# The last tile's gate on three column groups, and five first loads issued from ScalarE's queue

## The reference: windowed attention, a cosine layer, a routed expert layer

```python
# q, k, v: (4, 8, 576, 64); heads 0-3 see a window of 32 keys, heads 4-7 every 4th of 128
scores = where(mask, q @ k.T / 8, -1e9);  attn = softmax(scores);  x = attn @ v   # -> (2304, 512)
h = x @ w_in;  y = (h * cos(h)) @ w_out                        # (512, 2048), (2048, 512)
logits = y @ w_gate
noisy = logits + log1p(exp(y @ w_noise)) * noise               # (2304, 8)
# top 2 of 8 experts per row, softmax weights over the two
out[rows of e] += weight * (relu(y[rows] @ w1[e]) @ w2[e])      # (8, 512, 1024), (8, 1024, 512)
```

## Time and profile before

| | |
|---|---|
| runs | 1009.29, 1009.43, 1011.7 us; median 1009.43 us |
| profiled execution | 1009.55 us, span 1007.8 us |
| PE | 992.0 us busy, 98% of the span |
| DVE, ACT, POOL | 575.2, 445.8, 354.9 us busy |
| DMA | 101252 packets, 99.60 MB |

### The profile page before, as it was taken

The page is one execution under the profiler, slowest core; times in us unless marked ns, Lnnn a source line. Parts: engine busy times, 40 slices in busy tenths (PEclk is TensorE's granted clock), DMA queues, the critical chain, the costliest instruction groups (busy, mean ns, idle before and its releaser), DMA issues. The chain is left out here.

```text
span 1007.8 us, 17738 instructions
## 1 busy us (share of the span) xinstructions
PE 992.0 (98%) x6176; PEld 877.2 (87%) x6176; DVE 575.2 (57%) x1189; ACT 445.8 (44%) x1091; POOL 354.9 (35%) x349
## 2 busy tenths in 40 slices
PE   7999999999999999999999999999999999999998
PEld 5878898888889889889888888999898989999896
DVE  4888766576576576576676754434344444424322
ACT  5989665453454544534547333333132323323111
POOL 2656786222222222222231355143241425133241
PEclk9999999999999999999999999999999999999999
DMA  9787356000000000005006154434353533434130
GB/s 203 178 177 170 74 138 227 33 2 1 31 1 31 0 1 31 1 0 186 14 12 231 55 187 137 144 108 143 130 176 113 177 130 109 142 125 154 41 110 30
DMA packets 101252, 99.60 MB, mean 99 GB/s; under 512 B 72707, under 2 KB 73187, under 8 KB 101184
## 3 DMA queue, kind: packets, MB, share of 16 engines
q1 hardware_dynamic: 86352, 66.38, 22.2%
q0 software_dynamic: 10000, 31.15, 10.0%
q10 hardware_dynamic: 4832, 1.18, 0.7%
HBM read 80.61 MB, written 20.07 MB: 100 GB/s over the span
## 5 line engine op out<-in xcount | busy, mean ns | idle before, releaser
L1807 POOL TENSOR_TENSOR g_lo<-gate,g_hi 128x384 fp32r<-128x384 f32 x95 | 98.0, 1031 | 278.3 <-ACT g_hi L1099 278.3
L1159 ACT ACTIVATE uh_hi<-ps 128x306 fp32r<-128x306 f32 (+1 forms) x112 | 47.8, 426 | 274.1 <-PE ps L155 270.3
L154 PE MATMUL ps<-ux_lo,w_hi 128*128 128x306 f32 (+1 forms) x448 | 136.5, 305 | 0.0
L155 PE MATMUL ps<-ux_hi,w_hi 128*128 128x306 f32 (+1 forms) x448 | 136.0, 304 | 0.0
L153 PE MATMUL ps<-ux_hi,w_lo 128*128 128x306 f32 (+1 forms) x448 | 135.8, 303 | 0.1
L153 PE MATMUL ps<-x_hi,w_lo 128*128 128x384 f32 x384 | 133.6, 348 | 0.1
L1543 DVE SCALAR_TENSOR_TENSOR uh_lo<-ps,uh_hi 128x306 fp32r<-128x306 f32 (+1 forms) x112 | 53.3, 476 | 136.3 <-ACT uh_hi L1159 127.8
L155 PE MATMUL ps<-x_hi,w_hi 128*128 128x384 f32 x384 | 129.3, 337 | 0.0
L154 PE MATMUL ps<-x_lo,w_hi 128*128 128x384 f32 x384 | 129.2, 337 | 0.0
L153 PE MATMUL ps<-w_hi,g_lo 128*128 128x512 f32 x288 | 114.0, 396 | 0.5 <-DVE g_lo L1504 0.5
L155 PE MATMUL ps<-w_hi,g_hi 128*128 128x512 f32 x288 | 114.0, 396 | 0.0
(11 more groups left out here) (230 smaller groups left out, 2033.3 us busy)
## 6 DMA issues: line engine op xcount, KB each, us to landing
xT<-in_w SPq DMA_DIRECT2D x32, 1024.0 KB, 9.2
out<-table SPq DMA_DIRECT2D x18, 256.0 KB, 3.9
y_rows<-y_sb SPq DMA_DIRECT2D x6, 768.0 KB, 3.5
y_sb<-in_w_out SPq DMA_DIRECT2D x16, 256.0 KB, 3.4
q_raw<-in_q SPq DMA_DIRECT2D x40, 96.0 KB, 3.2
k_raw<-in_k SPq DMA_DIRECT2D x30, 96.0 KB, 2.8
w_raw<-in_w_in SPq DMA_DIRECT2D x4, 512.0 KB, 5.0
v_near<-in_v SPq DMA_DIRECT2D x8, 256.0 KB, 3.7
```

Of the source, the lines that this page charges most:

```text
L154: nc.tensor.matmul(psum, s_hi, m_lo, start=False, stop=False)
L155: return nc.tensor.matmul(psum, s_hi, m_hi, start=False, stop=stop)
L1159: nc.scalar.activation(u_h[0][:, f, piece_at[piece]], psH[:, f % 2, 0:PIECE[piece]], ACT.Relu).then_inc(u_hhi, 1)
L1807: nc.gpsimd.tensor_tensor(g2[1][:, f % 2, :], gate[:, f % 2, :], g2[0][:, f % 2, :], ALU.subtract).then_inc(glo_done, 1)
```

## The change

In attention, `load_v` and `load_w` become functions of the issuing engine. ACT issues `load_v(0, 1)` behind the k rows of step 4 (after `copy_q(0)`), `load_v(0, 2)` behind those of step 5 (after `copy_q(1)`), and `load_w(1)`, `(2)`, `(3)` at the ends of its steps 3, 6 and 9. SyncE no longer issues these. The last tile's three `gate_y`, with their three copies of logits, are replaced by `gate_all`, `copy_turned`, `turn_back` and `copy_all_logits`; the third transposed block and the turned result get places of their own behind `raw`. ACT's `first_part(0, 1)` moves behind the last `g_hi`; DVE's `last_low_g` moves ahead of `first_part(0, 0)` and `low_x(0)` ahead of `first_part(0, 1)`.

```diff
+        behind = xT[:].rearrange("p c s -> p (c s)")[:, QUANTA * QW:]
+        yT_end = yT + [behind[:, 0:DM].rearrange("p (d q) -> p d q", q=P)]
+        turned_end = behind[0:GN, DM:DM + P]
...
@@ SyncE
-            load_w(0)
-            load_v(0, 1)
+            load_w(sp, 0)
             load_qk(NT)
-            load_v(0, 2)
...
-                if s in (NT + 2, NT + 5, NT + 8):
-                    load_w((s - NT + 1) // 3)
@@ TensorE
             first_product(0, (1,))
-            gate_y(LAST, 0, 0)
             transpose_x(1)
-            gate_y(LAST, 1, 1)
+            gate_all(LAST)
             transpose_h(0, (0,))
-            gate_y(LAST, 2, 0)
+            turn_back(LAST)
             transpose_h(0, (1,))
@@ ScalarE, tile
-                    if last and f == FC - 1:
-                        first_part(0, 1)
                     act.wait_ge(g_done, m + 1)
...
                     nc.scalar.activation(g2[0][:, f % 2, :], gate[:, f % 2, :], ACT.Copy).then_inc(ghi_done, 1)
-                    if last and f == FC - 2:
-                        first_part(0, 0)
+                    if last and f >= FC - 2:
+                        first_part(0, f - FC + 2)
@@ ScalarE, attention
                 if s < 2:
                     load_rows(act, NT - 2 + s, k, k_raw)
+                    load_v(act, 0, s + 1)
...
+                if s in (3, 6, 9):
+                    load_w(act, s // 3)
@@ ScalarE, behind the last tile
-            copy_yT(LAST, 0, yT_last[0], yT[0])
-            copy_yT(LAST, 1, yT_last[1], yT[1])
-            copy_logits(LAST, 0)
-            copy_yT(LAST, 2, yT_last[2], yT[0])
+            for b in range(TB):
+                copy_yT(LAST, b, yT_last[b], yT_end[b])
             relu(0, 1)
-            copy_logits(LAST, 1)
             copy_x(1)
-            copy_logits(LAST, 2)
+            copy_turned(LAST)
+            copy_all_logits(LAST)
@@ VectorE
+            last_low_g()
             first_part(0, 0)
-            last_low_g()
+            low_x(0)
             first_part(0, 1)
-            low_x(0)
             first_part(1, 0)
             first_part(1, 1)
```

More of the change, by code:

```diff
@@ L393, in load_rows, with load_v, load_w @@
                 eng.dma_start(to[o:o + n, NH:H, :], dilated(src, b)[r, j:j + n, :, :]).then_inc(signal, 16)
+        def load_v(eng, b, g):
+            if b > 0:
+                eng.wait_ge(pv_done, NT * (b - 1) + g + GROUPS + 1)
+            near, p0 = v[b, 0:NH, :, :].rearrange("h (u s) d -> s (h u) d", u=2), WINDOW if g == 0 else 0
+            eng.dma_start(v_near[p0:P, g, :, :, :].rearrange("p h u d -> p (h u) d"),
+                         near[g * TQ - WINDOW + p0:(g + 1) * TQ]).then_inc(v_in_near[g], 16)
+            if g == 0:
+                eng.dma_start(v_near[0:WINDOW, g, :, 1, :],
+                             v[b, 0:NH, S // 2 - WINDOW:S // 2, :].rearrange("h s d -> s h d")
+                             ).then_inc(v_in_near[g], 16)
+            for t in (g, g + GROUPS):
+                for o, r, j, n in segments(t * TQ - WINDOW, TK):
+                    eng.dma_start(v_dil[o:o + n, t, :, :], dilated(v, b)[r, j:j + n, :, :]
+                                 ).then_inc(v_in_dil[t], 16)
+        def load_w(eng, j):
+            if j >= TB:
+                eng.wait_ge(wlo_done, 2 * (j - TB) + 2)
+            d, cols = w_chunk(2 * j)
+            eng.dma_start(w_raw[:, j % TB], w_in_v[:, d, cols.start:cols.start + 2 * WCH]
+                         ).then_inc(w_loaded[j % TB], 16)
         def w_chunk(n):
@@ L463, in _ @@
             sp.sem_inc(d_stored, 16)
[L465 to L479, removed]
             def load_qk(s):
@@ L485, in load_qk @@
                 load_rows(sp, s, k, k_raw)
[L487 to L493, removed]
             def load_ring(at, src):
@@ L516, in _ @@
                 if t == 3:
-                    load_v(0, 0)
-            load_w(0)
-            load_v(0, 1)
+                    load_v(sp, 0, 0)
+            load_w(sp, 0)
             load_qk(NT)
-            load_v(0, 2)
             for s in range(NT + 1, STEPS + GROUPS):
@@ L524, in _ @@
                 if b > 0 and t < GROUPS:
-                    load_v(b, t)
+                    load_v(sp, b, t)
                 if s < STEPS:
                     load_qk(s)
-                if s in (NT + 2, NT + 5, NT + 8):
-                    load_w((s - NT + 1) // 3)
                 if s == NT + 6:
@@ L697, in transpose_y @@
                 x.then_inc(tp_done, 1)
[L699 to L705, removed]
             def gate_all(i):
                 pe.wait_ge(tp_evac, TB * (i + 1))
+                y = yT_end if isinstance(i, int) and i == LAST else yT_all
                 for d in range(DC):
                     for b in range(TB):
-                        x = nc.tensor.matmul(ps_turned[GQ * b:GQ * (b + 1), :], wgn[:, d, 0:GQ], yT_all[b][:, d, :],
+                        x = nc.tensor.matmul(ps_turned[GQ * b:GQ * (b + 1), :], wgn[:, d, 0:GQ], y[b][:, d, :],
                                              start=(d == 0), stop=(d == DC - 1), skip_group_check=True)
@@ L718, in turn_back @@
                 pe.wait_ge(logits_out, TB * i + 1)
-                nc.tensor.transpose(ps_gate, turned, ident[0:GN, 0:GN]).then_inc(back_done, 1)
+                nc.tensor.transpose(ps_gate, turned_end if isinstance(i, int) and i == LAST else turned, ident[0:GN, 0:GN]).then_inc(back_done, 1)
             def rank(i):
@@ L1024, in copy_turned @@
                 act.wait_ge(gate_done, TB * (i + 1))
-                nc.scalar.activation(turned, ps_turned, ACT.Copy).then_inc(turned_out, 1)
+                nc.scalar.activation(turned_end if isinstance(i, int) and i == LAST else turned, ps_turned, ACT.Copy).then_inc(turned_out, 1)
             def copy_all_logits(i):
@@ L1030, in copy_all_logits @@
                                      ).then_inc(logits_out, TB)
-            def copy_logits(i, b):
-                act.wait_ge(gate_done, TB * i + b + 1)
-                nc.scalar.activation(logits[:, b, :], ps_gate[:, 0:2 * E], ACT.Copy).then_inc(logits_out, 1)
             def noise_exp(i):
```

## The result

The changed kernel takes 1013.96 us (median of 13 runs, 1012.27 to 1015.68) where the kernel before takes 1010.01 us (13 runs); the ratio is 1.0034, 95% interval 1.0025 to 1.0043. The forecast was +0.8 us and "within 0.3%"; it became about 4 us, slower by a hair more than that bound, and the time lies 0.4 us above the top of the range (the kernel before ran 0.5 us above its profiled execution in these runs, which is about that much). The profiled execution took 1014.01 us for a span of 1012.3, which is 4.46 us and 4.5 us more than before.

A forecast was written before the change was run, and what follows sets the result against it. PE, busy 98% of the span, was taken as the bound. ACT's issues +2.6 us, SyncE's relief -1.7 and the last tile -0.1 gave +0.8 on 1009.55: 1010.4 us, range 1007.4 to 1013.6.

The forecast's parts named there:

- Values on ScalarE's queue: Start of attention: ACT issuing two groups of values makes copy_q(3) 1.9 us late, and PE loses the same.
- The upper bound of 5.2 us: Start of attention: at 5 us a group on ACT's queue, copy_q(3) would be 5.2 us late.
- The prediction's own sign of being wrong: Wrong if copy_q(3) does not move or moves by 4 us, or if PE's k waits stay at 2.7 us.
- The rival of covered issues: Start: ACT's idle time covers all issues but the first weight piece, all k waits go; 1007.7 us, chance 0.20.
- The slow pace: Rival: a 2 us gap before scores(2) keeps PE slow through steps 4 and 5, 1.4 us each; 1013.2 us, chance 0.10.
- The slow drain: Rival at the start: ACT's queue needs 5 us a group, copy_q(2) later than about 18.5 us; 1013.7 us, chance 0.14.
- Weight pieces: ACT's steps 3, 6 and 9: issuing three pieces costs 0.45 us for the first and 0.2 us for the one in step 6.
- What SyncE gives back: Behind load_v(1, 0): k rows of steps 13 to 15 land earlier, 1.7 us of PE's waits won, bounds 0.5 and 2.7.
- the lower bound of 0.5: SyncE's lighter queue: only the 0.5 us of the one late weight piece at 57.62 us is won.
- Gate: Last tile: one gate_all and turn_back in place of three gate_y of 0.93 us each gain 1.35 us.
- Order: Last g: starts 0.46 us earlier, then PE waits about 0.44 us before each of three chunks; net loss 1.2 us.
- no hold-up: Behind the last g: the parts don't hold PE up at 533 us; 1.2 us better, 1009.2 us, chance 0.12.

The follow-up runs named there:

- first_values_in_the_idle: Kernel before with only load_v(0, 1) issued by ScalarE, behind step 5's k rows and ahead of copy_q(2): 1010.47 us against 1010.00, ratio 1.0002.
- the filled kernel: Changed kernel plus 9, 26 and 18 unread identity transposes in PE's waits before steps 2, 3 and the third scores product: 1015.59 us, before 1010.00.
- start_only: Kernel before with both groups of values and the three weight pieces issued by ScalarE, last tile unchanged: 1014.28 us against 1009.60, ratio 1.0043.
- values_only: Kernel before with only the two groups of values issued by ScalarE, weight pieces left on SyncE: 1014.58 us against 1009.60, ratio 1.0046.
- weights_only: Kernel before with only the three weight pieces issued by ScalarE: 1008.73 us against 1009.60, ratio 0.9992.
- order_only: Kernel before with only the new order at the last g, keeping the three gate_y: 1011.10 us against 1009.84, ratio 1.0007.
- tail_only: Kernel before with only the last tile's column-group gate and the new order of the last g, loads unchanged: 1009.35 us against 1009.60, ratio 1.0000.
- after_filled: Changed kernel plus 25 unread identity transposes in PE's waits of attention's steps 2 and 3: 1014.83 us, kernel before 1009.84, ratio 1.0050.
- warm_start: Kernel before plus 12 products of zeroed data on TensorE while it waits for its first rows: 1009.64 us against 1010.00, ratio 0.9996.
- gate_only: Kernel before with only the last tile's gate on three column groups, old order and loads kept: 1008.24 us against 1009.84, ratio 0.9984.

## Why the prediction was off, step by step

**Values on ScalarE's queue: right place, right mechanism, too small.** This is the step that failed by most: the duration taken for the two groups. The term was 1.9 us for a late `copy_q(3)`, with 0 and 5.2 as its bounds; measured, `copy_q(3)` is 3.97 us late. I had taken SyncE's own durations for the same transfers, 3.7 and 2.95 us; ACT's queue needed 4.9 and 4.1 us. The queue did drain slowly, as the rival had it; its mark, `copy_q(2)` later than about 18.5 us, was met by 0.1 us. In hindsight it should have had more than 0.14. One group alone on ACT's queue is nearly as slow, 4.3 us in first_values_in_the_idle, so the second group is not what makes the first one slow; why the same DMAs take longer on ACT's queue than on SyncE's is not shown. The upper bound of 5.2 us held. The prediction's own sign of being wrong, `copy_q(3)` moving by 4 us, was missed by 0.03 us. The rival of covered issues has a slip in its sum: it says that all waits for k rows go, which are 2.7 us, and takes off 2.2.

**The slow pace was no alternative to that but came on top.** I gave it as a rival of its own, worth 1.4 us a step for two steps. In the changed kernel's profile it is one step: step 4 is 5.06 us late where `copy_q(3)` is 3.97 late, 1.1 us more, and the filled kernel puts 1.4 us on it. In start_only and values_only it is two, as the rival had it: from step 4 to step 6 they need 9.79 and 9.99 us, the kernel before 8.06. Two rivals that share a cause (a late copy makes a gap, the gap keeps the pace low) should have been added, 3.97 + 1.1, and not set beside each other. The slow drain's 1013.7 us comes nearest to the measured time, in part by luck: it has 1.2 us too much for `copy_q(3)` and 0.65 us for the pieces, and lacks the slow pace and the 1.4 us that SyncE did not give back.

**Weight pieces: 0.65 us predicted, none found.** Between steps 4 and 6 PE needs 7.98 us, before 8.06. weights_only is no slower than before. The step that failed is the assumption that an issue at the end of an ACT step takes ACT's time: all three lie beside exponentials that go on unbroken.

**What SyncE gives back: 1.7 us predicted, 0.33 measured.** The step that failed is the assumption that the stall at 42.32 us was due to the weight piece in front. It is still there, 1.98 us long, with the piece gone. The text had named the right bound itself: the Trainium skill, "DMA: Bandwidth & Descriptors", section "Issuing engines are not separate DMA queues", says that spreading issues saves only the sequencer's time. The trace agrees: SyncE then stands from 37.27 to 44.74 us, and 0.33 us is left, against the lower bound of 0.5.

How much a lighter SyncE gives back depends on when PE gets there, and one profile of before is a weak yardstick for it. order_only and tail_only have before's loads; they reach step 6 at 26.75 and 26.78 us, wait 4.1 and 4.0 us for k rows (before: 2.7) and need 70.1 us from step 6 to the last. weights_only starts step 6 at 27.05 us and needs 68.16, 1.9 us less. With a late start the pieces make no such difference: values_only, with the pieces on SyncE, needs 67.69 us, and start_only, without them, 68.10. So these single profiles speak for the predicted 1.7 us where PE is early, and for nothing where the values have made it late, which is the case here.

**Gate: 1.35 us predicted, 1.66 in the changed kernel and 1.6 alone. Order: 1.2 us lost predicted, 1.27 and 1.3 measured,** with 0.46 us won at the last g as worked out. The gate's 0.3 us more are mostly `turn_back`, 0.10 us where I took 0.25, and the wait of 0.1 us that is not there. The waits were said to be 0.44 us for each chunk; the extra time for a chunk is 1.13 - 0.70 = 0.43. The rival "no hold-up" is out.

**The sum as measured in the two traces:** 5.06 (step 4) - 0.08 (to step 6) - 0.33 (to the last step) + 1.27 (order, on balance) - 1.66 (gate) = 4.26, the shift of `first_product(1)`; 4.28 at the wait for `h_lo`, 4.5 at the end. The last 0.2 us are not accounted for. I had put 0.19 on slower and 0.77 on no difference; with the measured ratio at 1.0034 the case lies at the border, and the error is one of size: about 2.1 + 1.1 us at the start and 1.4 us that SyncE did not give back, less 0.7 for the pieces and 0.3 for the tail: 0.8 + 2.1 + 1.1 + 1.4 - 0.7 - 0.3 = 4.4.

## What to carry to other kernels

A DMA on a compute engine's queue is paid for when the engine has nothing else to do while it is issued: count from the last thing that must be done to the next thing that is waited for, and take for each group what a full queue takes (here 4 to 5 us for 0.5 MB), not the half microsecond of a lone issue. Moved into an idle time that is long enough, five of the same DMAs were free within what can be told, and so were lone ones behind eight exponentials. A lead is only worth what the next shared resource lets through: 2.4 us won at the start ended in one wait for k rows at step 13, while 5 us lost went all the way to the end, because SyncE's next transfers wait for PE. When several edits share a change, time each: here two together helped by 2.4 us, one was worth minus 1.3 and one minus 5.

## What the runs showed of the hardware

*How long an issue blocks.* Four `v_dil` DMAs took ACT's queue 3.75 to 4.39 us and two took 3.56 to 4.27 us in the five kernels that have both groups there, while the k rows just ahead of them took 0.5 us each. The two at 14 us are the slower ones, 1.8 to 2.1 us for each.

*An issue beside activations.* A single weight piece took ACT's queue 0.33 to 0.38 us while ACT's exponentials went on at their usual distance, in the changed kernel and in weights_only, three times each.

*TensorE's pace after waits.* Behind waits of 1 to 3 us in attention the granted clock went to 0.50 to 0.77 for 5 to 10 us in values_only, start_only, after_filled and warm_start, and in gate_only at another place: PE waited 2.6 us for k rows at 61.55 us, and its windows then are

```profile
60.00:65.00 5.00, 3.45 (x22) 3.07 (x24) 1.92 (x5) 2.82 (x16) 1.89 (x1) 0.69 1.03 197
65.00:70.00 5.00, 5.00 (x49) 4.39 (x50) 2.85 (x8) 1.88 (x8) 0.33 (x1) 0.63 0.55 124
```

That execution took 1010.75 us, while the kernel's median is 1008.24. Not every such wait does it: in tail_only PE waited 1.98 us for k rows at 55.99 us, the granted clock stayed at 1.00 and the next scores product took 0.90 us. The Trainium skill, "TensorE: Matmul & The Clock Gate", Part 1, names two levels, half rate when idle and full rate when busy; these rows agree. What they add is that the column for the granted clock can miss it: in the changed kernel it reads 1.00 throughout the start, while the loads of the scores products take 1.68 us up to 24.7 us and 0.90 us from 27.6 us on. The pace is read from the durations of one operation.

*When the pace turns.* In kernels that are the same up to there it turned at about 18 us (before) and about 14 us (weights_only, gate_only, order_only and tail_only), with step 6 starting at 27.93 us and at 26.75 to 27.05 us. A difference of 1 us at the start of one profile is within that.
